# First attention group as four items of one batch each, without GpSimd, and Mish of unit 0 ahead of item 4

## What is computed

```python
for t in range(S):
    cur = einsum('bhd,bhe->bhde', u * k[t], v[t])
    y[t] = einsum('bhd,bhde->bhe', r[t], state + cur)
    state = w[..., None] * state + einsum('bhd,bhe->bhde', k[t], v[t])
x = y as (3072 tokens, 384)
h = x @ w_in;  g = h * tanh(log(1 + exp(h)));   x = g @ w_out      # Mish, 384 -> 2048 -> 384
h = x @ w_in2; g = where(h > 0, h, exp(h) - 1); out = g @ w_out2   # ELU
```

## Time and profile before

| | |
|---|---|
| median of 3 runs | 885.03 us (885.03 to 886.05) |
| profiled execution | 884.71 us, of which the span from first to last instruction is 883.2 us |
| mean granted TensorE clock | 0.992 |
| busy: TensorE / VectorE / ScalarE / GpSimd | 859.2 / 530.6 / 374.9 / 192.7 us |

### The profile page before, as it was taken

How to read it: one execution, slowest core, us unless ns; L and a number is a source line. 1 busy time by engine, 2 the same in 40 slices (tenths; PEclk the granted TensorE clock), 3 DMA queues, 4 the chain that set the end, 5 groups by cost and what they waited for, 6 DMA issues and landing times.

```text
span 883.2 us, 14651 instructions
## 1 busy us (share of the span) xinstructions
PE 859.2 (97%) x6480; PEld 709.3 (80%) x6480; DVE 530.6 (60%) x520; ACT 374.9 (42%) x374; POOL 192.7 (22%) x123
## 2 busy tenths in 40 slices
PE   6869999999999999999999999999999999999998
PEld 4758788888888888888878888888888888888886
DVE  7877877667777677753366754454454454455443
ACT  2286675567555666655888321121211211211211
POOL 7633344333444333410034500000000000000000
PEclk9979999999999999999999999999999999999999
DMA  7544432112221212302113410010010100000000
GB/s 268 173 143 128 143 98 97 52 61 99 102 61 70 78 53 91 118 2 81 54 49 95 144 36 1 36 36 1 36 36 1 36 1 0 36 1 1 36 0 37
DMA packets 19490, 57.20 MB, mean 65 GB/s; under 512 B 2912, under 2 KB 5344, under 8 KB 19424
## 3 DMA queue, kind: packets, MB, share of 16 engines
q1 hardware_dynamic: 14256, 45.43, 15.3%
q10 hardware_dynamic: 5168, 10.82, 3.5%
HBM read 44.44 MB, written 9.44 MB: 61 GB/s over the span
## 4 chain that ended last, share of the span: by engine, by line
PE 91%; ACT 2%; DVE 2%; DMA 1%; POOL 1%; issue 1%; SPq 0%; DVEq 0%; ACTq 0%
PE y_ps L720 43%; PE h_ps L668 31%; PE a_ps L668 11%; PE a_ps L553 2%; DMA att<-in_att 1%; PE a_ps L543 1%; PE a_ps L530 1%; PE y_ps L561 1%; ACT mid L856 0%; ACT mid L857 0%; DVE mid L984 0%; POOL att L234 0%; POOL att L348 0%; DVE g_lo L977 0%; DVE g_hi L975 0%
## 5 line engine op out<-in xcount | busy, mean ns | idle before, releaser
L668 PE MATMUL h_ps<-x_split,win_hi 128*128 128x512 f32 (+1 forms) x864 | 267.0, 391 | 0.9 <-ACT mid L857 0.5
L720 PE MATMUL y_ps<-g_hi,wout_hi 128*128 128x512 f32 x576 | 225.7, 392 | 8.2 <-DVE g_lo L977 7.0
L720 PE MATMUL y_ps<-g_hi,wout_lo 128*128 128x512 f32 x576 | 225.1, 391 | 0.0
L720 PE MATMUL y_ps<-g_lo,wout_hi 128*128 128x512 f32 x576 | 225.0, 391 | 0.0
L668 PEld LDWEIGHTS h_ps<-x_split,win_hi 128*128 128x128 f32 x864 | 160.6, 189 | 34.7 <-issue 1.2
L668 PE MATMUL h_ps<-x_split,win_lo 128*128 128x512 f32 (+1 forms) x432 | 167.3, 387 | 0.0
L984 DVE TENSOR_TENSOR mid<-mid 128x1024 f32<-128x1024 f32 x48 | 70.4, 1467 | 112.8 <-ACT mid L812 112.8
L977 DVE TENSOR_TENSOR g_lo<-mid,g_hi 128x1024 fp32r<-128x1024 f32 x96 | 134.1, 1397 | 3.3
L720 PEld LDWEIGHTS y_ps<-g_hi,wout_hi 128*128 128x128 f32 x576 | 108.8, 189 | 32.2 <-DVE g_lo L977 7.4
L720 PEld LDWEIGHTS y_ps<-g_hi,wout_lo 128*128 128x128 f32 x576 | 108.7, 189 | 22.8
L720 PEld LDWEIGHTS y_ps<-g_lo,wout_hi 128*128 128x128 f32 x576 | 108.9, 189 | 22.6
(11 more groups left out here) (115 smaller groups left out, 838.5 us busy)
## 6 DMA issues: line engine op xcount, KB each, us to landing
att<-in_att SPq DMA_DIRECT2D x22, 584.0 KB, 5.9
att<-in_att SPq DMA_DIRECT2D x22, 512.0 KB, 3.7
w_raw<-in_w_in SPq DMA_DIRECT2D x16, 384.0 KB, 4.1
w_raw<-in_w_out SPq DMA_DIRECT2D x16, 384.0 KB, 3.1
x_dram<-mid ACTq DMA_DIRECT2D x6, 768.0 KB, 3.4
att<-x_dram SPq DMA_DIRECT2D x6, 768.0 KB, 4.3
out<-mid ACTq DMA_DIRECT2D x5, 768.0 KB, 3.8
mid<-in_att SPq DMA_DIRECT2D x2, 584.0 KB, 8.6
```

The lines of the kernel that those rows point to most:

```text
L668: m = nc.tensor.matmul(ps, a, b_, start=n == 0, stop=n == len(terms) - 1)
L720: m = nc.tensor.matmul(y_ps[:, o, :], a, b_, start=unit == 0 and t == 0 and j == 0, stop=unit == UNITS - 1 and t == 1 and j == 2, skip_gro ...
```

## The change

Group 0 is cut differently: item n (0 to 3) is batch n with its first 128 times, instead of one chunk of 64 times of two batches. All of it goes without GpSimd and needs no state from an item before.

- Inputs: `first_T` (transposed keys and queries of 128 times) and `first_v` (values only); no natural keys and queries are loaded for items 0 to 3. T of item 0 and a small `u_cols` are issued from ScalarE's queue, T of item 1 first on SP's. `u` for the other items is loaded later, behind the third output.
- Powers: `pow_kr` is 128 columns wide, built by doubling to both sides at once from a reciprocal of 24 columns.
- Own scores (the term with u): VectorE multiplies keys by queries (512 columns), TensorE multiplies that by `u_side`, ScalarE copies the sums out and writes eight scaled copies of the identity into the score buffer; VectorE then copies what lies above the diagonal (in this layout) from PSUM over it.
- Natural keys: four transposes of the decayed keys on TensorE, one copy out of PSUM on ScalarE.
- GpSimd: nothing for items 0 to 3; it waits until the four decays are done, takes the decays and first products of items 4 and 5, zeroes the score buffers after the fourth output, and goes on as before.
- SP: order of loads changed; the gap copies of the first half are all issued by SP; weights 1 to 4 are loaded later in its list.
- VectorE's main loop: at V = 0 `mish(0)` runs ahead of `attention_after(0)` instead of behind it.
- The host puts the output's tokens in order accordingly.

The core of the diff:

```diff
@@ sync
             sp.dma_start(w_col[:, :], w).then_inc(pow_in, 16)
-            load_N(0)
-            load_T(0)
-            load_N(1)
-            load_T(1)
-            load_weights(0)
-            sp.wait_ge(mid_free, 1)
-            for n in (2, 3):
-                load_N(n)
-                load_T(n)
-                load_weights(n - 1)
-            fill_gaps(sp, 0, 0, heads=(0,))
-            load_weights(3)
+            load_first_T(1)
+            load_first_v(0)
+            load_first_v(1)
+            sp.wait_ge(mid_free, 1)
+            load_first_T(2)
+            load_first_T(3)
+            load_weights(0)
+            load_first_v(2)
+            load_first_v(3)
+            load_weights(1)
             load_chunk(4)
             load_chunk(5)
+            fill_gaps(sp, 0, 0)
+            sp.wait_ge(first_out_ps, 3)
+            sp.dma_start(u_all, u.partition_broadcast(128)).then_inc(u_in, 16)
+            load_weights(2)
             fill_gaps(sp, 0, 1, heads=(0,))
-            for j in range(4, len(W1_FIRST) + W_BUFS):
+            for j in range(3, len(W1_FIRST) + W_BUFS):
                 load_weights(j)
@@ gpsimd
-                own_product(0)
-                own_product(1)
-                decay_k(0)
-                decay_k(1)
-                for n in range(2, PER):
-                    own_product(n)
-                    decay_k(n)
+                pool.wait_ge(early_T, PER)
+                for n in (PER, PER + 1):
+                    decay_T(n)
+                    multiply_kr(n)
+                pool.wait_ge(first_out_ps, PER)
+                pool.memset(all_scores[:, :, :, :, :], 0.0).then_inc(masks, 1)
@@ tensor
+            def first_own(n):
...
+                for a in range(PAIRS):
+                    m = nc.tensor.matmul(y_ps[:, n % 2, 2 * a:2 * a + 2], kr_product[n % 2][:, a * ITEM:(a + 1) * ITEM],
+                                         u_side[:, a, :], start=True, stop=True, skip_group_check=True)
+            def first_item_scores(n):
+                pe.wait_ge(early_T, n + 1)
...
+                for p in range(PAIRS):
+                    for hh in range(2):
+                        m = nc.tensor.matmul(work_banks(n)[:, hh, p * ITEM:(p + 1) * ITEM], kr_T(n)[heads_rows(hh), 0, p, :],
+                                             kr_T(n)[heads_rows(hh), 1, p, :], start=True, stop=True, skip_group_check=True)
+            def first_keys(n):
...
+                for p in range(PAIRS):
+                    m = nc.tensor.transpose(h_ps[:, 0, p * ITEM:(p + 1) * ITEM], kr_T(n)[:, 0, p, :], ident)
-            keep_warm(10)
-            item_scores(0)
...
+            keep_warm(8)
+            first_own(0)
+            keep_warm(2)
+            first_item_scores(0)
+            first_keys(0)
+            first_own(1)
+            first_item_scores(1)
+            first_keys(1)
+            keep_warm(2)
+            first_main(0)
+            first_own(2)
+            keep_warm(2)
+            first_main(1)
+            first_item_scores(2)
+            first_keys(2)
+            first_own(3)
+            keep_warm(4)
+            first_item_scores(3)
+            first_keys(3)
+            first_main(2)
+            keep_warm(4)
+            first_main(3)
             pe.wait_ge(k_wide_done, 1)
@@ scalar
+            def first_own(n):
+                act.wait_ge(own_ps, n + 1)
+                act.activation(own[:, n % 2, :], y_ps[:, n % 2, 0:H], ACT.Copy).then_inc(own_done, 1)
...
+                for p in range(PAIRS):
+                    for hh in range(2):
+                        m = act.activation(first_scores[n % 2][:, hh, p, :], ident, ACT.Copy,
+                                           scale=own[:, n % 2, 2 * p + hh:2 * p + hh + 1])
+            def first_keys(n):
+                act.wait_ge(first_k_ps, n + 1)
+                act.activation(first_k(n), h_ps[:, 0, :], ACT.Copy).then_inc(first_k_done, 1)
...
+            first_own(0)
+            first_keys(0)
+            first_own(1)
+            first_keys(1)
+            first_x_hi(0)
+            first_own(2)
+            first_x_hi(1)
+            first_keys(2)
             weight_hi(0)
-            split_x_hi(0)
-            split_x_hi(1)
-            fill_gaps(act, 0, 0, heads=(1,))
+            first_own(3)
+            first_keys(3)
+            first_x_hi(2)
...
             weight_hi(1)
-            split_x_hi(2)
-            split_x_hi(3)
+            first_x_hi(3)
@@ vector
+            first_product(0)
+            decay_first(0)
+            first_product(1)
+            decay_first(1)
+            dve.wait_ge(consts, 5)
+            mask_first(0)
+            first_product(2)
+            decay_first(2)
+            mask_first(1)
+            first_x_lo(0)
...
+            first_state_of(0)
+            first_product(3)
+            decay_first(3)
+            first_x_lo(1)
+            first_state_of(1)
+            mask_first(2)
+            weight_lo(0)
+            mask_first(3)
+            first_x_lo(2)
+            first_state_of(2)
+            weight_lo(1)
+            first_x_lo(3)
+            first_state_of(3)
             dve.wait_ge(masks, MASKS)
             own_scores(PER)
             mask_scores(PER)
@@
                 elif V <= ALL:
                     if V > 0:
                         mish(V - 1)
+                    else:
+                        mish(V)
                     attention_after(V)
-                    if V < ALL:
+                    if 0 < V < ALL:
                         mish(V)
```

More of the change, by code:

```diff
@@ L27 @@
 LAG = 2
+LEVELS = 6
 ECOLS = 4
@@ L87, in attention_mlp @@
         att = [sb(f"att{i}", [128, A_COLS]) for i in range(2)]
[L88 to L93, removed]
+        all_scores, tables = sb("all_scores", [128, 2, 2, PAIRS, C]), sb("tables", [128, H * ITEM])
+        pow_kr = sb("pow_kr", [128, 2, PAIRS, ITEM])
+        state = sb("state", [128, COUPLES * KV_COLS + VPAD])
         causal, diagonal = sb("causal", [128, C]), sb("diagonal", [128, C])
         diag = sb("diag", [128, 2, H])
[L96 to L98 removed]
+        state_decay = sb("state_decay", [128, PAIRS])
+        neg_ln2, token = sb("neg_ln2", [128, 1]), sb("token", [1, 2])
         T = [mid[:, i * 1024:(i + 1) * 1024].rearrange("p (t n) -> p t n", t=2) for i in range(2)]
@@ L334, in _, with multiply_kr @@
             pool.memset(g_hi[0][:, 0, :].bitcast(f32), 0.0).then_inc(consts, 1)
[L335 to L340, removed]
+            pool.memset(state[:, :], 0.0).then_inc(state_zeroed, 1)
+            def multiply_kr(n):
                 i, count = loads_of(n)
@@ L898, in _ @@
-            m, at = 1, 0
-            while m < HALF:
+                return steps[0]
+            inside = k_powT[:, :, C - 1]
+            last = chain(dve.tensor_scalar(w_power[:, 1, 0, :], w_col, W_MIN, W_MAX, ALU.max, ALU.min))
+            dve.wait_ge(power_step, last)
+            for j in range(LEVELS - 1):
+                last = chain(dve.tensor_tensor(w_power[:, 1, j + 1, :], w_power[:, 1, j, :], w_power[:, 1, j, :], ALU.mult))
+                if j == 0:
+                    dve.tensor_tensor(inside, w_col, w_power[:, 1, 0, :], ALU.is_equal).then_inc(inside_step, 1)
+                    dve.wait_ge(inside_step, 1)
+                elif j == 1:
+                    dve.tensor_reduce(inside_min, inside, op=ALU.min, axis=AX.X).then_inc(inside_done, 1)
+                dve.wait_ge(power_step, last)
@@ L900, in _ @@
+            last = chain(dve.reciprocal(w_power[:, 0, :, :], w_power[:, 1, :, :]))
+            top = w_power[:, 1, LEVELS - 1, :]
+            chain(dve.tensor_tensor(state_decay[:, :], top, top, ALU.mult))
+            dve.wait_ge(power_step, last)
+            chain(dve.tensor_copy(r_powT[:, :, C - 1], w_power[:, 0, 0, :]))
+            last = chain(dve.tensor_tensor(k_powT[:, :, C], inside, w_power[:, 0, 0, :], ALU.mult))
+            for j in range(LEVELS):
+                m = 2 ** j
                 if m == 8:
@@ new lines, in _ @@
+                factor = w_power[:, :, j, :].unsqueeze(3).to_broadcast([128, 2, PAIRS, m])
+                swapped = w_power[:, ::-1, j, :].unsqueeze(3).to_broadcast([128, 2, PAIRS, m])
+                dve.wait_ge(power_step, last)
+                if m == HALF:
+                    dve.wait_ge(pow_done, 1)
+                if m == 1:
+                    chain(dve.tensor_tensor(first_decay, state_decay[:, :], top, ALU.mult))
+                last = chain(dve.tensor_tensor(pow_kr[:, :, :, C + m:C + 2 * m], pow_kr[:, :, :, C:C + m], factor, ALU.mult))
@@ new lines, in _, with first_product @@
+                op = dve.tensor_tensor(pow_kr[:, :, :, C - 2 * m:C - m], pow_kr[:, :, :, C - m:C], swapped, ALU.mult)
+                if 2 * m == HALF:
+                    op.then_inc(pow_done, 1)
+                else:
+                    last = chain(op)
+            dve.wait_ge(power_step, last)
+            def first_product(n):
+                dve.wait_ge(t_in[n], 16)
```

(4 more changed lines are left out.)

361 lines of the change are left out of this document (196 added, 165 removed).

## The result

| | before | after |
|---|---|---|
| median of 7 runs each | 885.03 us (882.8 to 886.39) | 880.72 us (876.74 to 881.74) |
| ratio after / before | | 0.9947, 95% interval 0.9927 to 0.9968 |
| profiled execution | 884.71, span 883.2 | 881.74, span 880.2 |
| busy TensorE / VectorE / ScalarE / GpSimd | 859.2 / 530.6 / 374.9 / 192.7 | 865.7 / 520.4 / 387.1 / 174.1 |

A forecast was written before the change was run, and what follows sets the result against it. TensorE was taken as one unbroken stream of matmuls, set by its first 60 us; 13.8 us earlier at the second second product, less 1.3 for an "issue" hole, net 12.5: median 872.5 us, range 868.5 to 879.

The forecast's parts named there:

- Part 1, Mish of unit 0: VectorE's Mish of unit 0 ahead of item 4: first second product 6.35 us sooner, 2.9 from full clock, 9.25 in all.
- rival 1: Clock falls in the hole before the first second product, which takes 7.0 us again: +2.4, 874.9 us; chance 0.2.
- the next common point is the second second product: Lay-out compared there: 57.6 us instead of 71.41, so 13.8 us earlier, taken as the gain before the allowance.
- Part 2, powers: Decay factors at the start on VectorE, with a new list of small operations: ready at 9.5 us, 8.99 before.
- Part 2, ScalarE's scaled copies: Eight 128-column copies per item in the first group, scaled by own scores: 0.29 us each, between 0.20 and 0.38.
- Part 2, TensorE: TensorE's pieces for each of items 0 to 3: 2.95 us per item, first product at 28.0 us.
- rival 3: Slower: TensorE does the first group's attention at 1.2 GHz, first product at 40.5 us or later, 888 us; chance 0.06.
- The prediction's own sign, a granted clock of 0.50 between 10 and 46 us: The prediction called itself wrong if the granted clock was 0.50 anywhere in that stretch.
- The allowance for a hole of "issue": One unexplained TensorE hole expected to remain, about at item 2 or 3: 1.3 us taken off the gain.
- The sum of 871.2: Forecast time if no hole of "issue" is due, by the skill page's rule of instruction refills.
- Weights and gap copies: Before unit 0: second half's gap copies land at 34.0 us, weights 3 and 4 split until 37.4, when Mish starts.
- one of the prediction's signs of being wrong: The prediction called itself wrong if the gap copies of the second half landed after 36 us.

The follow-up runs named there:

- e1: Kernel before with only Mish of unit 0 moved ahead of item 4 on VectorE; 880.05 us, ratio 0.9945.
- e3: Changed kernel with the low parts of the weights ahead of the next item's own scores on VectorE at odd V; 876.84 us, ratio 0.9902.
- e8: Changed kernel with SP issuing the next item's load ahead of the weights, VectorE's order left alone; 876.61 us, ratio 0.9902.
- e4: Changed kernel with 12 fillers instead of 8 ahead of the first own scores; 876.17 us, ratio 0.9902.
- e6: Changed kernel with 12 fillers and weights ahead of own scores at odd V, without the 14 fillers between pieces of items 0 to 3; 872.2 us, ratio 0.9867.
- e2: Changed kernel with Mish of unit 0 put back behind item 4, so the new start alone against the kernel before; 883.79 us, ratio 0.9991.
- e10: Changed kernel with Mish of unit 0 back behind item 4 and 12 fillers instead of 8; 880.22 us, ratio 0.9948.
- e7: Kernel before with Mish of unit 0 ahead of item 4 and weights ahead of own scores at odd V, old first group; 877.21 us, ratio 0.9911.
- e5: Changed kernel with 12 fillers instead of 8 and weights ahead of own scores at odd V; 872.41 us, ratio 0.986.

## Why the prediction was wrong

**Part 1, Mish of unit 0: right to 0.2 us where it was priced, wrong in what it is worth at the end.** Second product 9.37 us behind ScalarE's start (laid out 9.2); hole 1.5 (2.0), so rival 1 did not come true here; no fall of the clock, 4.1 us; distance to second product 2 11.2 (11.0). The failing step is "the next common point is the second second product": the lay-out ended there and the lead was carried to the end of the kernel. One product later the low part of the weights stands on VectorE behind own scores of item 7, which hang on GpSimd and on a load behind three others. Before, that chain was just hidden: the low part came in time for TensorE at 79.5, with a wait of 1.0 us only at the fifth product. The own scores of item 6 at its head hang on GpSimd, which the Mish move does not make earlier (it starts item 6 at 49.84 before and in e1), and the load of item 7 loses behind the weight loads most of what it is issued earlier. The lay-out named "item 6's own scores and three weight splits" as standing behind the moved Mish, and priced only the next Mish by it; it did not follow who waits for the splits: SP, then the load. e1, e3 and e8 show it: 5.4 us given back between second products 2 and 4, of which either edit returns 3.5 to 3.7. By e1 part 1 alone is worth 4.9 us, not 9.25 less 0.5.

**Part 2, powers: 1.0 us too long.** Laid out ready at 9.5, the first product of keys by queries started at 8.48. It gained nothing, as TensorE is the path from 9.22 on.

**Part 2, ScalarE's scaled copies: right.** Eight took 2.45 us, 0.31 each against 0.29.

**Part 2, TensorE: mis-sized.** At full clock (e4) own scores took 0.79 to 0.98 (laid out 0.45), scores 1.09 (0.85), transposes 0.59 (0.40), values 1.02 (0.85), keys by values 0.45 (0.40): about 4.0 per item instead of 2.95, and the 14 fillers 3.8 instead of 3.1. From 9.7 that gives 9.7 + 16.1 + 3.8 = 29.6, and 29.77 was seen, without a gap. The lay-out had VectorE and ScalarE as the path and TensorE waiting in between; with these terms TensorE is the path. This is 1.8 us, of which leaving the fillers out gives 1.2 back (e6).

**The clock at the start: rival 3, with a chance of 0.06, came true in half.** The prediction saw the eight fillers for ten, the hole and the short pieces, and set against them that a hole of 1.8 us leaves the clock at 1.00. That row speaks of a clock that had risen (first entry at 9.0); here it had not yet (21.1): that reading is the step that failed. Items 0 and 1 ran at 1.2 GHz, 5.2 us (34.97 less 29.77), not the whole stretch with 12.5. The prediction's own sign, a granted clock of 0.50 between 10 and 46 us, does not show in the view of this trace, for the reason given above; it does in e3 and e8. e2 beside e10 and the changed kernel beside e4 show it at the end too, 3.6 and 4.5 us.

**The allowance for a hole of "issue", 1.3 us: wrong.** The changed kernel and all runs with its first group have no such wait on TensorE; e1 and e7, with the old group, have them (the two longest 1.6 and 1.2; 2.1 and 1.5). The sum of 871.2, which goes by the Trainium skill, page "Runtime: NRT & Kernel Launch", section "Instruction fetch mechanics" (no such hole due), was the better one in this term for the new group. What these holes are in the old group stays open: no run took the instructions apart from the rest.

**Weights and gap copies: right in kind.** Laid out: Mish of unit 0 waits for weight 4, 9.4 us behind the first product's start; measured 8.4, behind ScalarE's split of that weight. The gap copies of the second half were issued from 35.58 on, took 2.2 to land, and so landed after 36, one of the prediction's signs of being wrong; that follows from the late first group.

The sum of what failed, at second product 2: laid out 57.6, measured 63.97, 6.4 us later, of which 5.2 clock, 1.8 TensorE's pieces, less 1.0 for the shorter wait for weight 4, and 0.2 each for the ways from unit 0 to second product 1 and from there to 2; and behind it 5.4 given back, 1.1 of it regained further on. Together that turns 13.8 into 3.0 in the profiled executions (4.3 by the medians). Where the 1.1 is regained was not taken apart. The kernel e5 took 872.41, where 872.5 was predicted. That is partly luck: it is 12.8 us ahead at second product 2 where 13.8 were laid out, its TensorE pieces are dearer, it still gives 2.4 back up to second product 4 and regains 2.1 behind it, and the 1.3 us taken off for a hole of "issue" had no hole to stand for.

## What to carry to other kernels

When a hole is closed, follow each engine's list past the next product to the step that was just in time behind it. Ask what does not come earlier with the rest (here GpSimd's work on item 6), what stands behind it in the next engine's list (three weight splits), who waits for those (SP), and what stands behind the waiter (the load of item 7). Lay-outs end when two consecutive rounds look the same as before, not at the first common point. And if work at a kernel's start moves from vector engines onto TensorE, price its pieces at both levels of its clock: filler matmuls that look like idle work may be what pays for the rest.

## What the runs showed of the hardware that was not expected

- Four more fillers on zeros ahead of the first work (12 for 8, 512 columns each) brought the first real matmuls from 1.2 to 2.4 GHz: scores of item 0 in 1.09 instead of 2.01 us, 5.2 us at the first product (e4 beside the changed kernel). In all five kernels with 12 fillers the first product came by 30.4.
- With eight fillers it was not the same in every execution. In e3 and e8 the first own scores took 1.05 (near full clock) and the transposes behind them again 1.04 and 1.05, so the clock rose and fell back: the view shows 0.50 in 14:18 in both. In the changed kernel and in e2 it did not rise until about 21 us. This may be why kernels with eight fillers vary so much (876.74 to 881.74, in e2 880.45 to 886.86); only one execution of each was traced.
- A low clock cost nothing where TensorE was not the path. In e7, with the old group and ten fillers, the view shows 0.69 in 10:14 and 0.88 in 14:18, and the first product came at 33.65 (33.69 before).
- Eight matmul records with 2 columns each, on fresh 128x128 weights, took 0.79 to 0.98 us, about 0.1 each. Four transposes with 128 columns each took 0.59, 0.15 each: so the columns are not what they cost. That the weight load is, is likely but not shown. The 64x64 pieces of the kernel before did 32 records in 0.69.
- VectorE and GpSimd reading SBUF at the same time: 3.29 us for a 1.23 us subtraction, by a lead of 0.3 us of the other (e4). With VectorE 0.3 us ahead (changed kernel) or 1.0 us (e5) it took 1.23. An earlier start can so cause a collision that a later one didn't have.
